# A spectral mixer with two feed-forward layers on one core: the layers run one after the other over all tokens, and layer 2's first product takes two token tiles together as seven block products

## The chip, the core and the metric

The kernel runs on one core of one Trainium2 chip. The metric is the device time of one execution in microseconds (us); less is better. TensorE (PE) multiplies matrices, PEld is its weight load; VectorE (DVE), ScalarE (ACT) and GpSimd (POOL) work element by element; SyncE (SP) issues the DMA transfers. Every engine runs its own list of instructions in order, and the lists are tied together by semaphores.

## The reference, cut to what matters

```
X = rfft(x, axis=1)                               # x: 2 x 3008 x 256, float32
Yr, Yi = complex product of X with w_r, w_i, + bias, then shrink by 0.01 towards 0
x = irfft(Yr + 1j*Yi, n=3008).reshape(6016, 256)
h = x @ moe_w_in;   x = (h * cos(h)) @ moe_w_out                  # 256 -> 2048 -> 256
h = x @ moe2_w_in;  out = (h * clip(h + 3, 0, 6) / 6) @ moe2_w_out
```

## The kernel before, in words

The first 190 us are the mixer: the transforms along the sequence as matmuls, with spills to HBM. The rest, about 1030 us, are the two feed-forward layers. 6016 tokens are 12 tiles: tile 0 has 384 tokens, the others 512. A tile is held as [128, 2, tokens]: two blocks of 128 features. The 2048 hidden features are taken as 8 pairs of two blocks of 128. One step G is one tile and one pair.

Every product is made of three matmuls, since TensorE reads rounded operands: high part of the weights by high part of the data, low by high, high by low. The high part is a rounding copy (`xh`, `gah`, `gbh`, `w1h`), the low part the difference (`xl`, `gal`, `gbl`, `w_lo`). So the first product of a step (`up`, L587) is 2 output blocks x 2 input blocks x 3 = 12 matmuls into two PSUM banks, and the second (`down`, L639) is 12 more, added up over the 8 pairs in two other banks.

Between the two, in layer 1, stands a chain of seven instructions on [128, 2, tokens], i.e. 1024 elements a partition: ACT `phase` (turns, L806), DVE `phase` (angle, L987), DVE `phase` (absolute value, a tensor_scalar that reads and writes SBUF, L991), ACT `cosine` (L814), DVE `ga` = h * cosine (L1009), ACT `gah` (L822), POOL `gal` (L1170). In layer 2 it is ACT `ramp` (L851), DVE `gb` (L1062), ACT `gbh` (L866), POOL `gbl` (L1176).

`feed_forward` runs both layers interleaved: step G of layer 1 and step G - 9 of layer 2 stand side by side in every engine's list (`pair`; `Live` says which parts are there), tiles 2 to 9 in a loop. The output of layer 1 goes from PSUM straight into layer 2's operands (`x2h`, `x2l`). On PE the order is up and down of layer 1, then up and down of layer 2, each `down` for the step before. There is one `phase`, one `ga` and one `gb` buffer. DVE splits the next tile's input into high and low part (L968, L973) in the last step of a tile; for tile 1 that is done in steps 5 and 6. The weights of layer 2 come in with the mixer's DMAs and are split in 16 pieces on ACT and POOL during tiles 0 and 1.

## Time and profile before

| | |
|---|---|
| median of 3 runs | 1220.2 us (1219.81 to 1221.41) |
| the profiled execution | 1220.21 us, of which 1218.4 us are the span from its first to its last instruction |
| PE busy | 1201.4 us (99%), 5576 matmuls |
| PEld, DVE, ACT, POOL busy | 1010.2, 605.7, 631.1, 559.9 us |
| granted TensorE clock, mean | 0.997 of full |
| DMA | 49.76 MB, mean 41 GB/s |

The profile page gives busy times by engine, a chain of waits that ended last, and groups of like instructions; the timeline gives single instructions with start, duration, and the idle time ahead of them. Matmuls are pipelined: one begins before the modelled end of the one before, so that their pace is read from start to start.

### The profile page before, as it was taken

The numbers are of one execution on the slowest core, as the hardware profiler recorded it, in microseconds if no ns is written. First come the engines' busy times: TensorE is split into PE (matmuls) and PEld (weight loads), VectorE is DVE, ScalarE is ACT, GpSimd is POOL, SyncE is SP. The second block draws the span as 40 slices with busy tenths as digits, with TensorE's granted clock in tenths as the row PEclk, the third lists the DMA queues.
The fourth block names the chain that finished last, engine by engine and source line by source line (L and its number), as shares of the span: only waits on it lengthen the run. The fifth ranks groups of instructions, "written<-read, shape, count | busy, mean of one in ns | idle before, by whom it ended". The sixth has DMA issues, their size and how long they took to land.

```text
span 1218.4 us, 14608 instructions
## 1 busy us (share of the span) xinstructions
PE 1201.4 (99%) x5576; PEld 1010.2 (83%) x5576; DVE 605.7 (50%) x599; ACT 631.1 (52%) x705; POOL 559.9 (46%) x294
## 2 busy tenths in 40 slices
PE   8999989999999999999999999999999999999998
PEld 8888789788888888888888888888888888888887
DVE  2787737645445435445354344444354454354344
ACT  2677656665544455445555445544455444554443
POOL 2577656675444443444434444344443444434410
PEclk9999989999999999999999999999999999999999
...
GB/s 251 139 247 230 130 137 115 18 1 1 31 1 1 35 1 0 34 0 29 5 0 34 0 0 34 0 0 34 0 0 34 0 0 34 0 1 18 1 18 18
DMA packets 26209, 49.76 MB, mean 41 GB/s; under 512 B 3185, under 2 KB 9969, under 8 KB 26024
## 3 DMA queue, kind: packets, MB, share of 16 engines
...
## 4 chain that ended last, share of the span: by engine, by line
PE 95%; DVE 2%; DMA 1%; ACT 1%; POOL 0%; issue 0%; SPq 0%; DVEq 0%; ACTq 0%
PE banks L587 41%; PE banks L639 41%; PE banks L492 2%; PE banks L507 2%; PE banks L508 2%; PE banks L512 2%; PE banks L565 2%; PE banks L528 1%; PE banks L527 1%; DMA v<-y_spill 1%; PE banks L477 0%; PE banks L543 0%; PE banks L540 0%; PE banks L541 0%; DVE phase L991 0%; DVE ga L1009 0%
## 5 line engine op out<-in xcount | busy, mean ns | idle before, releaser
L1170 POOL TENSOR_TENSOR gal<-ga,gah 128x1024 fp32r<-128x1024 f32 (+1 forms) x93 | 221.6, 2383 | 515.5 <-ACT gah L822 515.5
L987 DVE SCALAR_TENSOR_TENSOR phase<-phase,banks 128x1024 f32<-128x1024 int32 (+1 forms) x96 | 114.9, 1197 | 273.6 <-ACT phase L806 273.6
L1176 POOL TENSOR_TENSOR gbl<-gb,gbh 128x1024 fp32r<-128x1024 f32 (+1 forms) x88 | 206.6, 2348 | 16.6 <-ACT gbh L866 16.6
L814 ACT ACTIVATE cosine<-phase,half_pi 128x1024 f32<-128x1024 f32 (+1 forms) x96 | 109.1, 1136 | 192.7 <-DVE phase L991 192.1
L806 ACT ACTIVATE phase<-banks 128x1024 int32<-128x1024 f32 (+1 forms) x96 | 97.0, 1011 | 155.5 <-PE banks L587 154.9
L1009 DVE TENSOR_TENSOR ga<-banks,cosine 128x1024 f32<-128x1024 f32 (+1 forms) x96 | 115.4, 1202 | 104.9 <-ACT cosine L814 97.2
L1062 DVE SCALAR_TENSOR_TENSOR gb<-ramp,banks 128x1024 f32<-128x1024 f32 (+1 forms) x95 | 113.8, 1198 | 102.0 <-ACT ramp L851 101.9
L851 ACT ACTIVATE ramp<-banks,three 128x1024 f32<-128x1024 f32 (+1 forms) x95 | 104.3, 1098 | 109.0 <-PE banks L587 109.0
L866 ACT ACTIVATE gbh<-gb 128x1024 fp32r<-128x1024 f32 (+1 forms) x95 | 99.2, 1044 | 35.9 <-DVE gb L1062 31.6
L587 PE MATMUL banks<-xl,w1h 128*128 128x512 f32 (+1 forms) x384 | 116.6, 385 | 0.0
L587 PE MATMUL banks<-xh,w_lo 128*128 128x512 f32 (+1 forms) x384 | 116.6, 385 | 0.0
L587 PE MATMUL banks<-xh,w1h 128*128 128x512 f32 (+1 forms) x352 | 107.0, 385 | 0.0
L587 PE MATMUL banks<-x2h,w_lo 128*128 128x512 f32 (+1 forms) x352 | 106.8, 384 | 0.0
L587 PE MATMUL banks<-x2l,w2h 128*128 128x512 f32 (+1 forms) x352 | 106.7, 384 | 0.0
L587 PE MATMUL banks<-x2h,w2h 128*128 128x512 f32 (+1 forms) x352 | 106.7, 384 | 0.0
L822 ACT ACTIVATE gah<-ga 128x1024 fp32r<-128x1024 f32 (+1 forms) x96 | 99.2, 1034 | 10.6 <-DVE ga L1009 10.6
L639 PE MATMUL banks<-gah,w1h 128*128 128x512 f32 (+1 forms) x384 | 101.2, 385 | 1.9 <-ACT gah L822 1.9
L639 PE MATMUL banks<-gal,w1h 128*128 128x512 f32 (+1 forms) x384 | 101.7, 387 | 0.8 <-POOL gal L1170 0.6
L639 PE MATMUL banks<-gah,w_lo 128*128 128x512 f32 (+1 forms) x384 | 101.0, 385 | 0.0
L639 PE MATMUL banks<-gbh,w2h 128*128 128x512 f32 (+1 forms) x380 | 99.9, 385 | 0.0
L639 PE MATMUL banks<-gbh,w_lo 128*128 128x512 f32 (+1 forms) x380 | 99.8, 384 | 0.0
L639 PE MATMUL banks<-gbl,w2h 128*128 128x512 f32 (+1 forms) x380 | 99.8, 384 | 0.0
...
## 6 DMA issues: line engine op xcount, KB each, us to landing
w<-in_w_ff SPq DMA_DIRECT2D x32, 256.0 KB, 5.9
...
y_spill<-y SPq DMA_DIRECT2D x24, 256.0 KB, 2.2
xf<-x_spill SPq DMA_DIRECT2D x11, 512.0 KB, 4.3
...
out_y<-yt SPq DMA_DIRECT2D x10, 512.0 KB, 3.4
...
```

Of the source, the lines that this page charges most:

```text
L587: mm = pe.matmul(o, w[layer][:, at:at + P], a[:, c, 0:w_tok], start=(n == 0 and c == 0), stop=(n == 2 and c == DC - 1))
L639: mm = pe.matmul(bank[:, at_bank + c, 0:w_tok], w[layer][:, at:at + P], a[:, e, 0:w_tok], start=(p == 0 and n == 0 and e == 0), stop=(p == ...
L806: act.activation(phase[:, :, 0:w].bitcast(i32), bank[:, at:at + 2, 0:w], ACT.Copy, scale=1.0 / (2.0 * math.pi)).then_inc(a_turns, 1)
L814: act.activation(cosine[:, :, 0:w], phase[:, :, 0:w], ACT.Sin, bias=half_pi[:, :], scale=-1.0).then_inc(a_cos, 1)
L822: act.activation(gah[p % 2][:, :, 0:w], ga[:, :, 0:w], ACT.Copy).then_inc(a_gh, 1)
L851: act.activation(ramp[:, :, 0:w], bank[:, at:at + 2, 0:w], ACT.Relu, bias=three[:, :]).then_inc(b_ramp, 1)
L866: act.activation(gbh[pb % 2][:, :, 0:w], gb[:, :, 0:w], ACT.Copy).then_inc(b_gh, 1)
L987: dve.scalar_tensor_tensor(out=phase[:, :, 0:w], in0=phase[:, :, 0:w].bitcast(i32), scalar=-2.0 * math.pi, in1=bank[:, at:at + 2, 0:w], op ...
L1009: dve.tensor_tensor(ga[:, :, 0:w], bank[:, at:at + 2, 0:w], cosine[:, :, 0:w], ALU.mult).then_inc(a_g, 1)
L1062: dve.scalar_tensor_tensor(out=gb[:, :, 0:w], in0=ramp[:, :, 0:w], scalar=6.0, in1=bank[:, at:at + 2, 0:w], op0=ALU.min, op1=ALU.mult).the ...
L1170: pool.tensor_tensor(gal[p % 2][:, :, 0:w], ga[:, :, 0:w], gah[p % 2][:, :, 0:w].bitcast(fp32), ALU.subtract).then_inc(a_gl, 1)
L1176: pool.tensor_tensor(gbl[pb % 2][:, :, 0:w], gb[:, :, 0:w], gbh[pb % 2][:, :, 0:w].bitcast(fp32), ALU.subtract).then_inc(b_gl, 1)
```

## The change

Layer 1 now runs over all 12 tiles (96 steps, `up1(G)` followed by `down1(G - 2)`), and writes its output to HBM (`x2_spill`). Then layer 2 runs over 6 duos of two tiles (1024 tokens; the last duo has 2 x 448) and 8 pairs: 48 steps `step2`. There are two `phase` and two `ga` buffers now, and no loops: every step is written out.

In a step of layer 2 the hidden block is a 2x2 matrix of blocks (output block e by token tile), and so are the weights (A) and the data (B). In place of 8 block products there are 7 (`product`, three matmuls each, in order P1, P5, P2, P6, P3, P7, P4), on sums of blocks of the weights (`sum_w2`: S1 to S4, 4 instructions on 128x128 a pair) and of the data (`sum_t`: T1 to T4, 4 instructions on 128 x 512 a duo). P6 and P7 are added into the bank of P1, P3 into the bank of P5. ACT copies intermediate states out of PSUM (`u1`, `u5`, `u2`), and DVE adds them to what stands in a bank (`c11`, `c12`, `c22`). The fourth block, C21, stays in the bank. Ramp, `gb`, `gbh` and `gbl` are done block by block, 512 elements a partition in place of 1024, four of each a step; for three of the four DVE's `gb` has both operands in SBUF. The second product (`down2`) has 24 matmuls a step as before for two tiles. The seven data blocks of a duo are rounded and split (`round_t` on ACT, `t_low` on POOL) during the duo before; those of duo 1 in steps 5 to 7 of duo 0.

The split of the next tile's input in layer 1 moves from DVE to ACT (`round_x`, pair 3) and POOL (`x_low`, pairs 4 and 5), with two buffers. The weights of layer 2 are loaded and split for pairs 0 to 4 in tiles 2 to 6 of layer 1, for pairs 5 to 7 in the first steps of layer 2.

```diff
-STEPS_A = TILES * PAIRS
-LAG_B = PAIRS + 1
+STEPS1 = TILES * PAIRS
+DUOS = -(-TOKENS // (2 * TOK))
+LAST_W = (TOKENS - (DUOS - 1) * 2 * TOK) // 2
+STEPS2 = DUOS * PAIRS
+S1, S2, S4, A11, A12, A22, S3 = (i * P for i in range(7))
+UP2 = 7 * P
+W2COLS = UP2 + 2 * DIM
+EARLY = 5
+B11, B21, T3, B22, T1, T2, T4 = range(7)
...
+            def product(s, to, a, b, start, done):
+                q, p = divmod(s, PAIRS)
+                w = width2(q)
+                for n, (wt, x) in enumerate(((w2h, th), (w2l, th), (w2h, tl))):
+                    mm = pe.matmul(bank[:, to, 0:w], wt[p][:, a:a + P], x[q % 2][:, b, 0:w],
+                                   start=(start and n == 0), stop=(n == 2),
+                                   skip_group_check=not start)
+                mm.then_inc(done, 1)
+
+            def down2(s, i, c):
+                q, p = divmod(s, PAIRS)
+                e, tile = ((0, 0), (0, 1), (1, 1), (1, 0))[i]
+                count = 4 * s + i + 1
+                if c == 0:
+                    pe.wait_ge(b_gh, count)
+                    pe.wait_ge(b_gl, count)
+                if p == 0 and i == 0:
...
+                for n, (wt, a) in enumerate(((w2h, gbh), (w2l, gbh), (w2h, gbl))):
+                    mm = pe.matmul(bank[:, 4 + 2 * tile + c, 0:w], wt[p][:, at:at + P], a[block][:, 0:w],
+                                   start=(p == 0 and e == 0 and n == 0), stop=(p == PAIRS - 1 and e == 1 and n == 2))
+                if p == PAIRS - 1 and e == 1:
...
+            def step2(s):
+                q, p = divmod(s, PAIRS)
+                x = x_bank(s)
                 if p == 0:
-                    pe.wait_ge(xh_ready, t + 1)
-                    pe.wait_ge(xl_ready, t + 1)
-                if isinstance(G, int) and G <= LAG_B:
-                    if G >= 3:
-                        pe.wait_ge(a_g, G - 2)
-                    elif G == 2:
-                        pe.wait_ge(plus_done, GROUPS - 2)
-                        pe.wait_ge(c_copied, GROUPS - 2)
+                    pe.wait_ge(t_hi, 7 * (q + 1))
+                    pe.wait_ge(t_lo, 7 * (q + 1))
+                if q == 0:
+                    pe.wait_ge(w2_hi, 3 * (p + 1))
+                    pe.wait_ge(w2_lo, 2 * (p + 1))
+                    pe.wait_ge(w2_low_out, p + 1)
+                if s == 0:
+                    pe.wait_ge(a_g, STEPS1 - 2)
+                elif s >= 2:
+                    pe.wait_ge(b_g, 4 * (s - 1))
+                product(s, x, A11, B11, True, p1_done)
+                if s == 0:
+                    pe.wait_ge(a_g, STEPS1 - 1)
                 else:
-                    pe.wait_ge(a_g, G)
-                up(0, h_bank(G), p, x_hi(t), xl, step_width(G), a_h)
+                    pe.wait_ge(c12_done, s)
+                product(s, 2, S1, T1, True, p5_done)
+                if s >= 1:
+                    pe.wait_ge(c11_done, s)
+                product(s, 1, A12, B21, True, p2_done)
+                if s == 0:
+                    down1_half(STEPS1 - 2, 0)
+                else:
+                    down2(s - 1, 0, 0)
+                pe.wait_ge(u1_done, s + 1)
+                product(s, x, S2, T2, False, p6_done)
+                if s == 0:
+                    down1_half(STEPS1 - 2, 1)
+                else:
+                    down2(s - 1, 0, 1)
+                pe.wait_ge(u5_done, s + 1)
+                product(s, 2, S4, B22, False, p3_done)
+                if s >= 1:
+                    down2(s - 1, 1, 0)
+                pe.wait_ge(u2_done, s + 1)
+                product(s, x, S3, T3, False, p7_done)
+                if s == 0:
+                    down1_half(STEPS1 - 1, 0)
+                    down1_half(STEPS1 - 1, 1)
+                else:
+                    down2(s - 1, 1, 1)
+                    down2(s - 1, 2, 0)
+                    down2(s - 1, 2, 1)
+                pe.wait_ge(c22_done, s + 1)
+                product(s, x, A22, T4, False, p4_done)
...
+                up1(G)
                 if G == 2:
                     pe.wait_ge(plus_done, GROUPS)
                     pe.wait_ge(c_copied, GROUPS)
-                down_a(G - 2, G - 2)
-            feed_forward(pe, pair, PAIRS)
+                down1(G - 2)
+            for s in range(STEPS2):
+                step2(s)
...
+            for G in range(1, STEPS1 - 1):
+                take_cos(G)
+                take_turns(G + 1)
+                round_ga(G)
+                if G % PAIRS == 0:
+                    copy_x2(G // PAIRS - 1)
+                prepare1(G)
...
+            for s in range(STEPS2):
+                keep_u1(s)
+                keep_u5(s)
+                if s == 0:
+                    round_ga(STEPS1 - 1)
+                else:
+                    round_gb(s - 1, 3)
+                take_ramp(s, 0)
+                keep_u2(s)
+                round_gb(s, 0)
+                prepare2(s)
+                take_ramp(s, 1)
+                take_ramp(s, 2)
+                round_gb(s, 1)
+                round_gb(s, 2)
+                if s == 0:
+                    copy_x2(TILES - 1)
...
-            def take_ga(G, reuse):
+            def take_ga(G):
                 dve.wait_ge(a_cos, G + 1)
-                if reuse:
-                    dve.wait_ge(a_gh, G)
-                    dve.wait_ge(a_gl, G)
-                at, w = h_bank(G), step_width(G)
...
+                    dve.wait_ge(a_gh, G - 1)
+                    dve.wait_ge(a_gl, G - 1)
+                at, w = h_bank(G), width(G // PAIRS)
+                dve.tensor_tensor(ga[G % 2][:, :, 0:w], bank[:, at:at + 2, 0:w], cosine[:, :, 0:w], ALU.mult).then_inc(a_g, 1)
...
+            def take_c11(s):
+                w = width2(s // PAIRS)
+                dve.wait_ge(p2_done, s + 1)
+                dve.wait_ge(u1_done, s + 1)
+                dve.tensor_tensor(c11[:, 0:w], bank[:, 1, 0:w], u1[:, 0:w], ALU.add).then_inc(c11_done, 1)
...
+            def take_gb(s, i):
+                n, w = 4 * s + i, width2(s // PAIRS)
+                dve.wait_ge(b_ramp, n + 1)
+                if n >= G_BUFS:
+                    dve.wait_ge(b_gh, n - G_BUFS + 1)
+                    dve.wait_ge(b_gl, n - G_BUFS + 1)
+                h = (c11[:, 0:w], c12[:, 0:w], c22[:, 0:w], bank[:, x_bank(s), 0:w])[i]
+                dve.scalar_tensor_tensor(out=gb[n % G_BUFS][:, 0:w], in0=ramp[n % G_BUFS][:, 0:w], scalar=6.0,
+                                         in1=h, op0=ALU.min, op1=ALU.mult).then_inc(b_g, 1)
...
+            for G in range(1, STEPS1 - 1):
+                take_ga(G)
                 take_angle(G + 1)
-            feed_forward(dve, pair, PAIRS)
```

The list of DVE in layer 1, in the middle of a tile, before (`cosine_99` and the like are the program's names with buffer numbers):

```order
L987 SCALAR_TENSOR_TENSOR phase_116<-phase_116,banks 128x1024
L991 TENSOR_SCALAR phase_116<-phase_116 128x1024
L1009 TENSOR_TENSOR ga_96<-banks,cosine_99 128x1024
L1055 REGISTER_ALU
L1059 REGISTER_ALU
L1062 SCALAR_TENSOR_TENSOR gb_97<-ramp_129,banks 128x1024
```

And the same place in the changed kernel, two steps, where `ga1` is of the step before `phase0`:

```order
L1164 TENSOR_TENSOR ga1_132<-banks,cosine_102 128x1024
L1142 SCALAR_TENSOR_TENSOR phase0_100<-phase0_100,banks 128x1024
L1146 TENSOR_SCALAR phase0_100<-phase0_100 128x1024
L1164 TENSOR_TENSOR ga0_103<-banks,cosine_102 128x1024
L1142 SCALAR_TENSOR_TENSOR phase1_101<-phase1_101,banks 128x1024
L1146 TENSOR_SCALAR phase1_101<-phase1_101 128x1024
```

The `gb` of layer 2 no longer stands between one step's `ga` and the next step's angle: the angle follows `ga` directly. In the same way ACT's list of layer 1 is now:

```order
L885 ACTIVATE cosine_102<-phase1_101,half_pi_62 128x1024
L877 ACTIVATE phase0_100<-banks 128x1024
L893 ACTIVATE gah1_105<-ga1_132 128x1024
L885 ACTIVATE cosine_102<-phase0_100,half_pi_62 128x1024
L877 ACTIVATE phase1_101<-banks 128x1024
```

where it was, in the same stretch:

```order
L806 ACTIVATE phase_116<-banks 128x1024
L814 ACTIVATE cosine_99<-phase_116,half_pi_62 128x1024
L851 ACTIVATE ramp_129<-banks,three_63 128x1024
L822 ACTIVATE gah0_120<-ga_96 128x1024
L866 ACTIVATE gbh1_125<-gb_97 128x1024
```

The turns of step G + 1 moved from behind to ahead of the rounding `gah` of step G, and the two instructions of layer 2 are gone from between. PE's list in layer 2, before, is one step of one tile:

```order
L587 MATMUL banks<-x2h,w2h 128x512 x2
L587 MATMUL banks<-x2h,w_lo 128x512 x2
L587 MATMUL banks<-x2l,w2h 128x512 x2
L587 MATMUL banks<-x2h,w2h 128x512 x2
L587 MATMUL banks<-x2h,w_lo 128x512 x2
L587 MATMUL banks<-x2l,w2h 128x512 x2
L639 MATMUL banks<-gbh_124,w2h 128x512 x4
L639 MATMUL banks<-gbh_124,w_lo 128x512 x4
L639 MATMUL banks<-gbl_126,w2h 128x512 x4
```

and in the changed kernel, here P2, a `down2` half, P6 and the next half of a step:

```order
L664 MATMUL banks<-th0_130,w2h4_128 128x512
L664 MATMUL banks<-th0_130,w2_4_lo_142 128x512
L664 MATMUL banks<-t0_lo_144,w2h4_128 128x512
L684 MATMUL banks<-gbh4_175,w2h3_127 128x512
L684 MATMUL banks<-gbh4_175,w2_3_lo_140 128x512
L684 MATMUL banks<-gbl4_176,w2h3_127 128x512
L664 MATMUL banks<-th0_130,w2h4_128 128x512
L664 MATMUL banks<-th0_130,w2_4_lo_142 128x512
L664 MATMUL banks<-t0_lo_144,w2h4_128 128x512
L684 MATMUL banks<-gbh4_175,w2h3_127 128x512
L684 MATMUL banks<-gbh4_175,w2_3_lo_140 128x512
L684 MATMUL banks<-gbl4_176,w2h3_127 128x512
```

The products now come in groups of three matmuls, of this step's first product and the last step's second by turns, where 12 stood together.

## Rows read from the trace of the kernel before

**Rows 1.** The page: busy times, and the chain that ended last by engine.

```profile
PE 1201.4 (99%) x5576; PEld 1010.2 (83%) x5576; DVE 605.7 (50%) x599; ACT 631.1 (52%) x705; POOL 559.9 (46%) x294
...
PE 95%; DVE 2%; DMA 1%; ACT 1%; POOL 0%; issue 0%; SPq 0%; DVEq 0%; ACTq 0%
```

**Rows 2.** The chain of waits in order of time: start, duration, what.

```profile
249.14 2.10 PE banks L587 x12
251.24 2.08 PE banks L639 x12
...
350.08 2.72 PE banks L587 x12
```

**Rows 3.** Timeline of PE where tile 1 begins; idle time in brackets.

```profile
213.90 0.98 PE L639 MATMUL banks<-gal,w1h 128*128 128x384 f32 x4
...
220.97 0.98 PE L639 MATMUL banks<-gah,w1h 128*128 128x384 f32 x4 [0.83 <-ACT gah L822]
...
227.07 1.17 PE L639 MATMUL banks<-gah,w1h 128*128 128x512 f32 x4 [0.45 <-ACT gah L822]
...
233.70 0.74 PE L587 MATMUL banks<-yt_lo,w1h 128*128 128x512 f32 x2 [0.93 <-DVE ga L1009]
```

**Rows 4.** Timeline of PE in the mixer: start, duration, what (21 matmuls apart).

```profile
79.88 0.39 PE L507 MATMUL banks<-wmh,uh 128*128 128x512 f32 x1
...
84.64 0.39 PE L507 MATMUL banks<-wmh,uh 128*128 128x512 f32 x1
```

**Rows 5.** Groups by form: busy, mean ns of one, idle before.

```profile
L845 ACT ACTIVATE ramp<-banks,three 128x512 f32<-128x512 f32 x2 | 1.4, 689 | 1.3 <-PE banks L587 1.3
L1075 DVE TENSOR_TENSOR gbl<-gb,gbh 128x512 fp32r<-128x512 f32 x2 | 1.4, 688 | 0.1
L1126 POOL TENSOR_TENSOR w_lo<-w,w1h 128x512 fp32r<-128x512 f32 x5 | 6.3, 1266 | 7.0 <-ACT w1h L754 7.0
```

**Rows 6.** The page's DMA issues: what, count, KB each, median us to landing.

```profile
xf<-x_spill SPq DMA_DIRECT2D x11, 512.0 KB, 4.3
```

**Rows 7.** Timelines of ACT, DVE and POOL in tile 0 and where tile 1 begins.

```profile
198.50 0.56 DVE L991 TENSOR_SCALAR phase<-phase 128x768 int32<-128x768 int32 x1
198.56 2.20 POOL L1170 TENSOR_TENSOR gal<-ga,gah 128x768 fp32r<-128x768 f32 x1 [2.05 <-ACT gah L822]
219.08 0.96 DVE L1009 TENSOR_TENSOR ga<-banks,cosine 128x768 f32<-128x768 f32 x1 [1.83 <-POOL gal L1170]
219.96 1.21 DVE L987 SCALAR_TENSOR_TENSOR phase<-phase,banks 128x1024 f32<-128x1024 int32 x1
220.99 1.84 POOL L1170 TENSOR_TENSOR gal<-ga,gah 128x768 fp32r<-128x768 f32 x1 [0.79 <-ACT gah L822]
221.20 2.18 DVE L991 TENSOR_SCALAR phase<-phase 128x1024 int32<-128x1024 int32 x1
224.61 1.23 DVE L1009 TENSOR_TENSOR ga<-banks,cosine 128x1024 f32<-128x1024 f32 x1 [1.22 <-ACT cosine L814]
225.87 1.06 ACT L822 ACTIVATE gah<-ga 128x1024 fp32r<-128x1024 f32 x1 [0.60 <-DVE ga L1009]
227.00 2.40 POOL L1170 TENSOR_TENSOR gal<-ga,gah 128x1024 fp32r<-128x1024 f32 x1 [2.47 <-ACT gah L822]
```

**Rows 8.** Timeline of all engines, one step of layer 1 in the loop.

```profile
555.18 1.22 DVE L987 SCALAR_TENSOR_TENSOR phase<-phase,banks 128x1024 f32<-128x1024 int32 x1 [3.90 <-ACT phase L806]
556.44 0.69 DVE L991 TENSOR_SCALAR phase<-phase 128x1024 int32<-128x1024 int32 x1
557.17 1.15 ACT L814 ACTIVATE cosine<-phase,half_pi 128x1024 f32<-128x1024 f32 x1 [2.02 <-DVE phase L991]
558.36 1.22 DVE L1009 TENSOR_TENSOR ga<-banks,cosine 128x1024 f32<-128x1024 f32 x1 [1.22 <-ACT cosine L814]
```

**Rows 9.** Stretches: length, busy by engine, granted clock, DMA share, GB/s.

```profile
156.00:158.00 2.00, 2.00 (x9) 2.00 (x10) 0.00 (x0) 0.07 (x1) 1.72 (x2) 0.50 0.36 74
```

**Rows 10.** Timeline of PE: its longest idle time after the start.

```profile
155.86 2.04 PE L565 MATMUL banks<-c2s,v 120*128 120x120 f32 x8 [4.04 <-DMA v<-y_spill]
```

More of the change, by code:

```diff
@@ new lines, in mixer_program @@
+        r = Region(work_at)
+        for p in range(EARLY):
+            w2f[p], w2l[p] = twice(r, f"w2_{p}", [P, W2COLS])
+        tf[0], tl[0] = twice(r, "t0", [P, 7, TOK])
+        assert r.at <= nc.sbuf_usable_end
+        r = Region(w1_at)
+        c11, c12, c22 = r.place("c11", ONE, fp32), r.place("c12", ONE, fp32), r.place("c22", ONE, fp32)
+        u1, u2 = r.place("u1", ONE, fp32), r.place("u2", ONE, fp32)
+        ramp = [r.place(f"ramp{i}", ONE, fp32) for i in range(2)]
+        assert r.at <= w1_at + 4 * PCOLS * 4
@@ L177, in mixer_program @@
+        gbh, gbl = [], []
+        r = Region(u_at)
+        for i in range(RING):
+            at = r if i < RING - 1 else spare
+            gbh.append(at.place(f"gbh{i}", ONE, f32r))
+            gbl.append(at.place(f"gbl{i}", ONE, f32r))
+        assert spare.at <= small_at and r.at <= phase_at + 2 * TOK * 4
+        th[1] = r.place("th1", [P, 7, TOK], f32r)
+        tf[1], tl[1] = twice(r, "t1", [P, 7, TOK])
+        assert r.at <= v_at
         bank = ctx.enter_context(nc.psum_tensor("banks", [P, 8, 512], fp32))
@@ L700, in _ @@
[L700 to L701 removed]
+                    up1(1)
+            for G in range(2, STEPS1):
+                up1(G)
                 if G == 2:
```

955 lines of the change are left out of this document (558 added, 397 removed).

## The prediction

> **What bounds the kernel now.** The page comes first: PE is busy 99% of the span and stands in 95% of the chain that ended last [rows 1]; no other engine is over half busy except ACT at 52%. From 234 us on the chain of waits alternates 12 matmuls of L587 and 12 of L639 without a gap. So a matmul taken away there is worth its pace, as long as PE is not made to wait. The pace: 12 matmuls of 512 columns take 2.72 us, of 384 columns 2.10 (first product) or 2.08 (second) [rows 2]. That is 0.2267 and 0.1733 to 0.175 us each; a column is (0.2267 - 0.1733)/128 = 0.417 ns, and 448 columns come to 0.200 us. Only the beginning of tile 1 shows feed-forward time lost: between the starts at 213.90 and 233.70 [rows 3] PE issued 36 matmuls of 512 columns and 40 of 384, 8.2 + 6.9 = 15.1 us of work in 19.8 us.
>
> **The change, part by part.**
>
> First product of layer 2. Before: 11 tiles x 8 pairs x 12 = 1056 matmuls at 0.2267 and 96 at 0.175, 256.2 us. After: 21 a step, 40 steps at 0.2267 and 8 steps at 0.200, 190.4 + 33.6 = 224.0 us. **-32.2 us.** The second product: 256.0 before; after 40 x 24 x 0.2267 + 8 x 24 x 0.200 = 256.0. Zero.
>
> The seven waits of a step's products and eight of its second products break PE's list into threes. In the mixer 21 matmuls of mixed lines, with groups of two to six and about as many satisfied waits, go from 79.88 to 84.64 [rows 4], 0.2267 each. A satisfied wait costs nothing; taken at zero, without an upper bound of its own.
>
> Is every wait of a layer-2 step satisfied when PE comes to it? A step is 45 x 0.2267 = 10.20 us, a product 0.68. Half-size work costs 0.69 on ACT and DVE, 1.27 on POOL [rows 5] (copies are nearer 0.6; I take 0.60 to 0.63). Busy: ACT 11 x 0.65 = 7.1, DVE 7 x 0.69 = 4.8, POOL 4 x 1.27 = 5.1. The handoffs, from the step's start, PE's results seen some 0.2 after a group (a matmul's 0.39 less its pace, [rows 4]): u1 0.9 to 1.5, wanted by P6 at 2.72; u5 to 2.2, wanted at 4.08; c11 to 3.0, ramp 3.7, u2 4.3, wanted by P7 at 5.44; c12 5.7, P7 seen at 6.3, c22 7.0, wanted by P4 at 8.16. The least slack is 1.1 us. The low parts are wanted a step later. ACT's roundings for the next duo stand behind these (two a step, 1.3 us, in a hole); the w2 pieces of steps 2 to 4 too. Zero, upper bound in the rivals.
>
> Duo 1 is the exception: POOL has in step 7 four `gbl` and four `t_low`, and step 8 needs all 14 low parts. Counting from step 7: the last `gbl` of step 6 ends at 4.1, then five instructions to 4.1 + 5 x 1.29 = 10.5, against 10.2; with three `gb` of DVE that hold POOL up (below) some 0.5 each, 12.0. **+1.7 us**, from 0.3 to 2.5.
>
> Start of tile 1. The split leaves DVE, comes three pairs ahead, and `w2` pieces no longer stand between. All of 19.8 - 15.1 comes back: **-4.7 us**, from -2 to -5.
>
> Turn from layer 1 to layer 2. The last cosine stands ahead of u1, u5, the last `gah`, ramp and u2 on ACT, and the last `ga` behind c11 on DVE. From the end of the last `up1`: cosine ends at 6.4 (held up as below), u1 at 7.0, where P6 could begin at 6.1; `ga` to 8.9, `gah` 9.95, ramp 10.6, u2 11.2, where P7 could begin at 9.8. **+2.4 us**, from 0.5 to 3.5.
>
> The extra transfers (`x2` out and in again, about 12 MB), the sums for pairs 0 to 4 and duo 0, and `x2` copied by ACT lie under layer 1, whose DMA queue is nearly idle. On SP's queue six loads of w2 for pairs 5 to 7, the last spill of `x2` and the two loads of duo 1 wait for layer 1's end, one behind the other. At 4.3 us for 512 KB [rows 6] pair 5 is there 4 to 9 us later and all of it within 26; DVE asks for pair 5 at the end of step 1, some 10 us later, and for duo 1 at the end of step 4, some 40. Hidden; if pair 5 came 5 us later than this, DVE's c11 would wait in step 2, and PE with it. A tile's end: `x2` is out 1.0 us after the last `down1` is seen, under an `up1` of 2.72. Zero.
>
> **Layer 1 alone, where this is decided.** PE's step is now 24 x 0.2267 = 5.44 us; before it was 10.88, which hid everything. The chain that cannot be doubled up runs from the end of one `ga` to the end of the next. On DVE the angle starts 0.08 before `ga` ends (219.96 against 219.08 + 0.96), and the absolute value 1.24 after the angle's start [rows 7]: 1.16 after `ga`'s end. On the other side `gah` and then `gal`: 227.00 against 225.84, also **1.16** [rows 7]. From the absolute value's start to the end of `ga` are 3.14 us (556.44 to 558.36 + 1.22) [rows 8]. Now the two collide, as twice in [rows 7]. At 198.50 the absolute value started 0.06 first, took its 0.56, and `gal` took 2.20 where alone it takes 1.84. At 220.99 `gal` started 0.21 first, and the absolute value took 2.18 against 0.69 [rows 7, 8] and ended 0.55 after it. One waits for the other's end.
>
> If the absolute value goes first: 1.16 + 3.14 = 4.30 us a step, under 5.44. If `gal` goes first: 1.16 + 2.40 + 0.55 + (3.14 - 0.69) = 6.56 us, over it.
> When the chain is ahead of PE, turns wait for PE; then `gah` follows the turns (they stand ahead of it) and `gal` starts about 0.25 before the absolute value, and wins. That step ends with `ga` 2.0 us after the next step's turns could begin. In the step after that, `gah` waits for `ga`, and the tie of 1.16 decides. Won: `ga` ends 0.9 after PE's time, the chain is ahead again, and the two kinds alternate at PE's pace; the late `gal` ends 11.6 us after its turns began, wanted at 12.5. No wait. Lost: every step of 512 tokens takes 6.56, 88 x 1.12 = +98.6 us. In tile 0 (768 elements) the absolute value leads by 0.06, so it isn't decided there.
> I take it as won. Rows of 0.01 us can't part 1.16 from 1.16; but the angle directly behind `ga` is a bit shorter than after a pause (1.21 [rows 7] against 1.22 [rows 8]), and `gal` is at 1.16 with a `gah` after a pause, as it will be; so the absolute value should be the first by some 0.005 to 0.01.
> The Trainium skill ("SBUF — State Buffer", Who interferes with whom) says that DVE in a two-port mode, or with two inputs in SBUF, and GpSimd take a shared pair of ports as an exclusive lock, and that whoever issues first has it for the whole instruction. On the lock the trace agrees (2.18 against 0.69), and on who gets it too, for leads of 0.06 and 0.21. At 1.16 against 1.16 the rule gives 1187 or 1286 and cannot choose.
>
> **Sum.** Against the span of 1218.4: -32.2 - 4.7 + 1.7 + 2.4 = 1185.6; with the 1.8 us around the span 1187.4. The profiled execution (1220.21) is the median of the runs (1220.2), so no correction: **1187.4 us**. With the bounds of the terms 1184 to 1193.
>
> **Rivals.**
> 1. *The tie is lost* (slower). Place: absolute value L1146 behind `gal` L1344, every step of tiles 1 to 11. It decides as soon as the chain is over 5.44, i.e. when `gal` wins nearly all ties; price +98.6, time 1286. For it: nothing but 0.01 us stands against it, and POOL may ask for its port sooner or later than its start shows. Against it: both rows go to the one that started first. Should PE's idle time of 1.1 us in each step also lower its clock, it is more. The clock fell to 0.50 [rows 9] after idle time of 4.04 us [rows 10]; whether pauses of 1.1 would do it no row shows. I take no loss.
> 2. *Some ties are lost, or layer 2's handoffs miss.* A won tie takes back 1.14 us and a lost one adds 1.12, and `gal` has 0.9 to spare: with a third lost PE waits now and then. Or in layer 2 `gb` with both operands in SBUF collides with `gbl`, 0.3 to 0.5 us each, more than the 1.1 of slack when two meet ahead of u2 or c22; 0.3 us too much in 48 steps are 14 us. Time 1197 to 1217.
> 3. *The start of tile 1 isn't won back and the turns cost their upper bounds*: 1187.4 + 4.7 + 1.9 = 1194. Within the forecast's edge.
> 4. *No change* needs losses of just 32 us: no mechanism gives that but a share of lost ties.
>
> **How the numbers follow.** The forecast (1183 to 1197) gets 0.60, rival 2 0.12, rival 1 0.25, the rest 0.03, most of it between 1217 and 1275. The forecast's own range is 1183 to 1197. As rival 1 alone holds more than 2 in 10, the range reaches to it: 1182 to 1290. A measurement of this kernel tells 0.2% (2.4 us) from no change. Faster: 0.60 + 0.12 + 0.01 = 0.73; within 0.2%: 0.01; slower 0.26.
>
> **What would show it.** 1008 matmuls in `product`, 1152 in the second product, at 0.2267. In layer 1 starts of `up1` 5.44 apart, and durations of the absolute value that alternate between 0.69 and about 2.7; if rival 1 holds, all of them are long, steps are 6.56 apart, and PE waits for `gal`. One idle time of 1 to 2 us where step 8 of layer 2 begins, and two at the turn ahead of P6 and P7. No pause at 213 us. Steps of layer 2 are 10.20 apart. Wrong would be the forecast if the absolute values are all long, or if PE waits for u2 or c22 in the middle of a duo.

## The result, and the profile after

The changed kernel takes **1198.5 us** (median of 4 runs, 1196.6 to 1199.44), the kernel before 1220.3 beside it: a ratio of 0.9818 (95% interval 0.9801 to 0.9835). That is 21.8 us or 1.8% faster. The forecast was 1187.4 us, so 11.1 us too low. The measured time lies in the stated range of 1182 to 1290 only because that range reaches out to rival 1; it is 1.5 us above the forecast's own range (1183 to 1197), and in that of rival 2 (1197 to 1217).

The page of the changed kernel, its busy times and its chain by engine, against [rows 1]:

```profile
PE 1171.4 (98%) x5432; PEld 986.6 (82%) x5432; DVE 790.7 (66%) x839; ACT 777.5 (65%) x1100; POOL 754.2 (63%) x493
...
PE 91%; DVE 3%; DMA 2%; ACT 2%; issue 2%; POOL 0%; SPq 0%; DVEq 0%; ACTq 0%
```

PE is 30 us less busy, but the span is only 20.7 us shorter (1218.4 to 1197.7), and PE's share of the chain fell from 95% to 91%. Part of the gain went into waits.

The place that the prediction called decisive is the pair of the absolute value (DVE, L1146) and `gal` (POOL, L1344). The timeline of the two, two steps late in layer 1, with the idle time ahead in brackets:

```profile
682.11 2.39 POOL L1344 TENSOR_TENSOR gal<-ga,gah 128x1024 fp32r<-128x1024 f32 x1 [1.37 <-ACT gah L893]
682.38 2.68 DVE L1146 TENSOR_SCALAR phase<-phase 128x1024 int32<-128x1024 int32 x1
688.67 0.69 DVE L1146 TENSOR_SCALAR phase<-phase 128x1024 int32<-128x1024 int32 x1
688.68 2.95 POOL L1344 TENSOR_TENSOR gal<-ga,gah 128x1024 fp32r<-128x1024 f32 x1 [4.17 <-ACT gah L893]
```

In one step `gal` starts 0.27 ahead and the absolute value takes 2.68; in the next the absolute value starts 0.01 ahead, takes 0.69, and `gal` takes 2.95. All 88 steps of 512 tokens follow this alternation: 44 ties, each won by DVE with a lead of 9 to 16 ns. PE notices nothing. Its timeline where steps of layer 1 begin shows them 5.44 apart:

```profile
557.47 0.62 PE L625 MATMUL banks<-xh,w1h 128*128 128x512 f32 x2
...
562.91 0.62 PE L625 MATMUL banks<-xh,w1h 128*128 128x512 f32 x2
```

So layer 1 went as predicted. The loss stands in the first duo of layer 2. PE's timeline there: the first matmul of P1 of steps 3, 4, 5, 6, 7 and 8 (727.33, 738.31, 750.66, 765.09, 775.29, 788.28), with the first of P7 in steps 3 to 5 ("issue" means that the profile shows no releaser):

```profile
727.33 0.39 PE L664 MATMUL banks<-th,w2h 128*128 128x512 f32 x1
...
733.41 0.50 PE L664 MATMUL banks<-th,w2h 128*128 128x512 f32 x1 [0.48 <-ACT u L1002]
...
738.31 0.39 PE L664 MATMUL banks<-th,w2h 128*128 128x512 f32 x1
...
745.76 0.50 PE L664 MATMUL banks<-th,w2h 128*128 128x512 f32 x1 [1.85 <-ACT u L1002]
...
750.66 0.39 PE L664 MATMUL banks<-th,w2h 128*128 128x512 f32 x1
...
758.56 0.50 PE L664 MATMUL banks<-th,w2h 128*128 128x512 f32 x1 [2.30 <-ACT u L1002]
...
765.09 0.39 PE L664 MATMUL banks<-th,w2h 128*128 128x512 f32 x1
...
775.29 0.39 PE L664 MATMUL banks<-th,w2h 128*128 128x512 f32 x1
...
788.28 0.47 PE L664 MATMUL banks<-th,w2h 128*128 128x512 f32 x1 [2.63 <-issue]
```

The prediction has 10.20 for a step. Steps 3 to 5 take 10.98, 12.35 and 14.43: 7.2 us more in all, and P7 waits for `u2` (ACT L1002) in each. Step 7 takes 12.99 and step 8 10.28, 2.9 us more, because P1 of step 8 waits (2.63 of idle time; counted from start to start it is 2.8 over the pace). Steps 0 and 1, the turn from layer 1, take 12.51 and 11.15, 3.3 us more. Steps 2 and 6 and all steps 9 to 39 take 10.20.

The timeline of POOL, DVE and ACT around step 4 (begun at 738.31) shows why `u2` is late:

```profile
735.60 2.73 POOL L1366 TENSOR_TENSOR w_lo<-w,w2h 128x448 fp32r<-128x448 f32 x2
736.37 2.51 DVE L1191 SCALAR_TENSOR_TENSOR gb<-ramp,c 128x512 f32<-128x512 f32 x2 [1.27 <-ACT ramp L1017]
...
740.15 0.69 DVE L1191 SCALAR_TENSOR_TENSOR gb<-ramp,banks 128x512 f32<-128x512 f32 x1 [1.27 <-ACT ramp L1017]
740.76 0.68 DVE L1207 TENSOR_TENSOR w<-w 128x128 f32<-128x128 f32 x1
741.47 0.29 DVE L1209 TENSOR_TENSOR w<-w 128x128 f32<-128x128 f32 x1
741.68 0.28 DVE L1210 TENSOR_TENSOR w<-w 128x128 f32<-128x128 f32 x1
742.00 1.26 DVE L1212 TENSOR_TENSOR w<-w 128x128 f32<-128x128 f32 x1
743.19 0.68 DVE L1216 TENSOR_TENSOR w_lo<-w,w2h 128x512 fp32r<-128x512 f32 x1
743.79 0.68 DVE L1170 TENSOR_TENSOR c<-banks,u 128x512 f32<-128x512 f32 x1
744.50 0.72 ACT L1017 ACTIVATE ramp<-c,three 128x512 f32<-128x512 f32 x1 [2.89 <-DVE c L1170]
745.13 0.58 ACT L1002 ACTIVATE u<-banks 128x512 f32<-128x512 f32 x1
```

Five instructions that prepare the weights of later pairs, 3.0 us, stand between `gb` 3 and `c11`. `c11` begins 5.5 us after the step's start, where it begins at 2.24 in steps 9 to 39; ACT's ramp waits 2.89 for it, and `u2` stands behind the ramp. The 3.0 us are not all of it: `gb` 3 itself ends 2.5 after the step's start (0.3 to 1.5 in steps 9 to 39). Ahead of it two `gb` took 2.51 for the pair beside POOL's low parts of w2. In step 2, 1.9 us of DVE's preparation stand at the same place behind a `gb` 3 that ends at 0.4, and `c11` still begins at 2.24.

In step 5 the wait has a second price. Stretches of 3 us each in and behind P7's wait (length, busy by engine, granted clock, DMA share, GB/s):

```profile
755.00:758.00 3.00, 1.26 (x6) 0.72 (x4) 2.16 (x3) 0.70 (x2) 0.32 (x1) 1.00 0.00 0
758.00:761.00 3.00, 2.44 (x7) 1.98 (x8) 1.98 (x3) 2.73 (x7) 1.29 (x1) 0.72 0.00 0
761.00:764.00 3.00, 3.00 (x11) 2.32 (x11) 1.30 (x2) 2.02 (x5) 1.47 (x2) 0.71 0.00 0
```

After the wait of 2.30 the granted clock is 0.72 and 0.71 on average; eight matmuls start 0.43 apart in place of 0.227, i.e. at 1.2 GHz, and cost 1.6 us more. That makes step 5 the longest.

### The profile page after: what moved, and what is told of

Its sections match the earlier page's. It is cut to its first block, busy times and chain, and to the rows that moved or that the text cites. A ratio compares the mean times of both kernels' runs of the same rounds, so it can differ in the third digit from the quotient of the medians.

```text
span 1197.7 us, 15354 instructions
## 1 busy us (share of the span) xinstructions
PE 1171.4 (98%) x5432; PEld 986.6 (82%) x5432; DVE 790.7 (66%) x839; ACT 777.5 (65%) x1100; POOL 754.2 (63%) x493
## 4 chain that ended last, share of the span: by engine, by line
PE 91%; DVE 3%; DMA 2%; ACT 2%; issue 2%; POOL 0%; SPq 0%; DVEq 0%; ACTq 0%
PE banks L625 21%; PE banks L642 21%; PE banks L684 20%; PE banks L664 17%; PE banks L539 2%; PE banks L534 2%; PE banks L535 2%; PE banks L592 1%; PE banks L519 1%; PE banks L555 1%; PE banks L554 1%; DVE gb L1191 1%; DMA xb<-in_x 1%; DMA v<-y_spill 1%; ACT ramp L1017 1%
## 5 line engine op out<-in xcount | busy, mean ns | idle before, releaser
L1344 POOL TENSOR_TENSOR gal<-ga,gah 128x1024 fp32r<-128x1024 f32 (+1 forms) x95 | 249.5, 2626 | 177.8 <-ACT gah L893 176.3
L1424 POOL TENSOR_TENSOR gbl<-gb,gbh 128x512 fp32r<-128x512 f32 (+1 forms) x192 | 248.1, 1304 | 176.0 <-ACT gbh L1024 176.0
L1191 DVE SCALAR_TENSOR_TENSOR gb<-ramp,c 128x512 f32<-128x512 f32 (+1 forms) x144 | 126.1, 881 | 50.9 <-ACT ramp L1017 50.9
L1146 DVE TENSOR_SCALAR phase<-phase 128x1024 int32<-128x1024 int32 (+1 forms) x96 | 156.7, 1632 | 3.3
L1024 ACT ACTIVATE gbh<-gb 128x512 fp32r<-128x512 f32 (+1 forms) x192 | 118.7, 619 | 50.8 <-DVE gb L1191 50.7
L684 PE MATMUL banks<-gbh,w_lo 128*128 128x512 f32 (+1 forms) x384 | 148.6, 387 | 0.0
L664 PE MATMUL banks<-th,w2h 128*128 128x512 f32 (+1 forms) x336 | 130.1, 387 | 9.0 <-ACT u L1002 5.7
L1017 ACT ACTIVATE ramp<-c,three 128x512 f32<-128x512 f32 (+1 forms) x144 | 101.9, 712 | 50.0 <-DVE c L1170 21.1
L664 PE MATMUL banks<-t_lo,w2h 128*128 128x512 f32 (+1 forms) x336 | 129.4, 385 | 0.0
L664 PE MATMUL banks<-th,w_lo 128*128 128x512 f32 (+1 forms) x336 | 129.4, 385 | 0.0
L1142 DVE SCALAR_TENSOR_TENSOR phase<-phase,banks 128x1024 f32<-128x1024 int32 (+1 forms) x96 | 114.6, 1193 | 9.7 <-ACT phase L877 9.7
L625 PE MATMUL banks<-x_lo,w1h 128*128 128x512 f32 (+1 forms) x384 | 116.5, 385 | 0.0
```

Source lines behind the costliest of these rows:

```text
L625: mm = pe.matmul(o, wt[:, at:at + P], a[:, c, 0:w], start=(n == 0 and c == 0), stop=(n == 2 and c == DC - 1))
L664: mm = pe.matmul(bank[:, to, 0:w], wt[p][:, a:a + P], x[q % 2][:, b, 0:w], start=(start and n == 0), stop=(n == 2), skip_group_check=not s ...
L684: mm = pe.matmul(bank[:, 4 + 2 * tile + c, 0:w], wt[p][:, at:at + P], a[block][:, 0:w], start=(p == 0 and e == 0 and n == 0), stop=(p == P ...
L1017: act.activation(ramp[n % G_BUFS][:, 0:w], h, ACT.Relu, bias=three[:, :]).then_inc(b_ramp, 1)
L1024: act.activation(gbh[n % RING][:, 0:w], gb[n % G_BUFS][:, 0:w], ACT.Copy).then_inc(b_gh, 1)
L1142: dve.scalar_tensor_tensor(out=angle[:, :, 0:w], in0=angle[:, :, 0:w].bitcast(i32), scalar=-2.0 * math.pi, in1=bank[:, at:at + 2, 0:w], op ...
```

## The experiments

The times are medians of 4 to 9 runs, in the two runs on the tie of 2; the kernel before had 1220.3 to 1220.4 beside all of them. Steps are those of layer 2 unless said otherwise. "The changed kernel" is the one of the case.

### `u2` ahead of the ramp

```diff
-                take_ramp(s, 0)
                 keep_u2(s)
+                take_ramp(s, 0)
```

> Edit: on ACT, u2 stands ahead of ramp 0 in every step of layer 2 (nothing else moved). Theory A: in steps 3 to 5 of layer 2 P7 waits for u2 because u2 stands behind ramp 0, which waits for c11, and c11 stands on DVE behind the preparation of w2 and of duo 1; those steps lost 0.8 + 2.1 + 4.2 = 7.2 us over 10.20. With u2 first P7 waits for nothing; c22, still late on DVE, holds P4 by some 0.6 and 1.0 us in steps 4 and 5. Steps 3 to 5 lose 1 to 2.5 us in place of 7.2, and the turn to layer 2 gives 0.6 back: about 1193 us (1191 to 1195) against 1198.5 of the changed kernel. Rival B: those steps are bound by ACT or POOL's amount of work (roundings and low parts of w2), so that the order of two instructions moves the loss to another wait: 1197 to 1199.

Measured: 1199.1 us, ratio 0.9828 (0.9814 to 0.9841). No gain. The waits of PE in this kernel, from 690 to 800 us (in total, times, longest):

```profile
PE banks L664 <- ACT u L988: 3.1, 4, 1.0
PE banks L664 <- issue: 3.1, 1, 3.1
PE banks L664 <- DVE c L1182: 2.1, 2, 1.3
...
PE banks L664 <- ACT u L1002: 0.5, 1, 0.5
```

`u2` (L1002) now costs 0.5, at the turn alone, where it cost 5.7. But P4 waits for `c22` (L1182) in steps 4 and 5, P6 for `u1` (L988) in steps 4, 5 and 7, and P1 of step 8 waits longer. Steps 4, 5 and 7 take 12.3, 12.8 and 14.8. The low clock stands elsewhere here: it did not fall in step 5 but behind the wait ahead of step 8 (0.63 from 787 to 790), which took 11.91. Rival B's time and its moved waits held. Its reason, the amount of ACT's or POOL's work, did not: the next run moves only DVE's work, and most of the loss goes. Another order on ACT only changes which product meets the late `c11`.

### DVE's preparation moved away from `c11`

```diff
                 take_c22(s)
+                prepare2(s)
                 take_gb(s, 1)
...
                 take_gb(s, 3)
-                prepare2(s)
```

> Edit: DVE's preparation in layer 2 (sums and low parts of w2, sums of the next duo's blocks) moves from behind gb 3, where c11 of the next step stands behind it, to between c22 and gb 1. Theory A (the amount of DVE's work ahead of c11 makes u2 late): c11 of steps 3 to 5 begins 3.0 to 3.6 us after the step's start in place of 4.1 to 5.9, and of the 7.2 us 0.5 to 2.5 are left: about 1193 us. Rival B (POOL's low parts of w2, which hold gb back on the shared port: two gb took 2.51 us in place of 1.30, push gb 3 and c11 late by themselves): about half of the loss stays, 3 to 4 us: 1195 to 1196. Duo 1's stall of 2.8 us at step 8 stays in both, perhaps 0.3 us more.

Measured: 1193.8 us, ratio 0.9782 (0.9769 to 0.9796), as theory A had it. Steps 3, 4 and 5 take 10.20, 11.11 and 11.57: 2.3 of the 7.2 us are left. The same table of PE's waits:

```profile
...
PE banks L664 <- ACT u L988: 2.3, 3, 1.1
PE banks L664 <- ACT u L1002: 1.1, 1, 1.1
...
```

P7's waits in steps 3 to 5 are gone; the remainder is P6's for `u1`, which stands on ACT behind `gbh` 2 and ramp 3. Steps 7 and 8 (2.6 over) and the turn stayed, as both theories had it. With the same instructions in another place, their place ahead of `c11` is shown as the cause of 4.9 of the 7.2 us (steps alone; 1.6 of it is the low clock of step 5, which didn't come). The rest is the lateness of the `gb`: `c11` of steps 4 and 5 still begins 3.6 and 4.0 after the step's start, directly behind `gb` 3.

### The tie, tried with one short instruction

```diff
                 take_ga(G)
+                dve.memset(pause[:, :], 0.0)
                 take_angle(G + 1)
```

> Edit: in layer 1 DVE clears one element a partition between each ga and the next angle, some 0.06 us. In the trace of the changed kernel every second absolute value begins 9 to 16 ns ahead of gal and takes 0.69 us; with the edit it begins after it. Theory (prediction, rival 1): whoever starts first has the port, so every absolute value of 1024 elements takes about 2.7, a step of layer 1 is 6.56 us long in place of 5.44, 88 steps make +98.6 us: about 1297 us (1285 to 1310); more if PE's clock falls with its pauses of 1.1 us. Rival: the lock isn't decided by 0.06 us of order, or the ring has slack: the alternation stays and the time is 1198 to 1200.

Measured: 1199.5 us, ratio 0.9829 (0.9811 to 0.9848). The clearing overlapped with `ga` and moved the absolute value by only some 14 ns. Timeline of one such tie:

```profile
438.35 2.95 POOL L1346 TENSOR_TENSOR gal<-ga,gah 128x1024 fp32r<-128x1024 f32 x1 [2.47 <-ACT gah L894]
...
438.36 0.69 DVE L1147 TENSOR_SCALAR phase<-phase 128x1024 int32<-128x1024 int32 x1
```

The record of `gal` begins first here, and DVE still has the port. The 44 ties lie between 5 ns behind and 3 ns ahead, and DVE won them all. The edit was too small to test the price, and it shows that the margin is larger than the 9 to 16 ns.

### The tie, lost

```diff
                 take_ga(G)
+                for n in range(3):
+                    dve.memset(pause[:, 32 * n:32 * n + 32], 0.0)
                 take_angle(G + 1)
```

> Edit: as in the run with one small clearing, but three clearings of 32 elements a partition stand between ga and the next angle in layer 1. One clearing moved the start of the absolute value by only some 14 ns (44 ties between 5 ns behind gal and 3 ns ahead of it, all still won by DVE: 0.69 us), so it did not test the rule. Three should put it 0.05 to 0.2 us behind gal. Theory (rival 1 of the prediction): from there on gal has the port first in every step of 1024 elements, the absolute value takes 2.7 to 2.9 us, the ring is 6.56 us, 88 x 1.12 = +98.6 us: about 1297 us (1285 to 1310). Rival: the port isn't given by the order of the starts but by something else (DVE wins all ties below 0.1 us): 1198 to 1201 and the alternation stays.

Measured: 1303.3 us, ratio 1.0679 (1.066 to 1.0699). Timeline of DVE and POOL, two steps in a row:

```profile
501.66 2.40 POOL L1347 TENSOR_TENSOR gal<-ga,gah 128x1024 fp32r<-128x1024 f32 x1 [1.79 <-ACT gah L894]
501.73 2.87 DVE L1147 TENSOR_SCALAR phase<-phase 128x1024 int32<-128x1024 int32 x1
...
508.22 2.39 POOL L1347 TENSOR_TENSOR gal<-ga,gah 128x1024 fp32r<-128x1024 f32 x1 [2.60 <-ACT gah L894]
508.30 2.86 DVE L1147 TENSOR_SCALAR phase<-phase 128x1024 int32<-128x1024 int32 x1
```

0.07 behind is enough: `gal` goes first in every step, the absolute value takes 2.87, and the steps are 6.56 apart, the number of the prediction. Layer 2 begins 100 us later (793.7 against 693.5); the turn adds 3.5. So 0.17 us of clearings cost 105 us: rival 1 was real in mechanism and price, and a shift of 0.08 us is enough to get there. The granted clock over layer 1 stayed at 1.00: PE waited in pieces of 0.2 and 0.4 us, and of 0.6 and 1.1 at the ends of tiles. Layer 1 took 99.3 us more against 98.6 in the prediction, but not quite as priced: 4.3 of it stand in tile 0, where the clearings turned the lead of 0.06 into 0.03 behind, and 95.0 in tiles 1 to 11. One of the steps of tile 0 (768 elements, 0.56 us when it goes first):

```profile
200.89 1.84 POOL L1347 TENSOR_TENSOR gal<-ga,gah 128x768 fp32r<-128x768 f32 x1 [3.34 <-ACT gah L894]
200.92 2.23 DVE L1147 TENSOR_SCALAR phase<-phase 128x768 int32<-128x768 int32 x1
```

The Trainium skill ("SBUF — State Buffer", Who interferes with whom) gives the port to whoever issues first. At 0.07 and at 0.03 us this run agrees; at a few ns the records of the run before don't tell who issued first.

### An eighth block product

```diff
+                product(s, 1, A12, B21, True, None)
                 product(s, 1, A12, B21, True, p2_done)
```

> Edit: P2 is computed twice in each step of layer 2 (three matmuls more, eight block products; the result is the same). Theory (price of a block product is its pace, since PE bounds layer 2): 40 x 3 x 0.2267 + 8 x 3 x 0.2027 = 32.1 us more; steps 3 to 5 and the turn have 0.68 us more cover ahead of P7 each and lose some 2.5 us less: +29.5 us, about 1228 us (1226 to 1231), so slower than the kernel before. Rival: PE has hidden slack in layer 2 (engines other than PE set the step), then +10 or less.

Measured: 1224.6 us, ratio 1.0037 (1.0024 to 1.0051): slower than the kernel before, and 26.1 over the changed kernel, less than the 29.5 of the theory. Steps 9 to 39 take 10.88, exactly 0.68 more. But steps 0 to 8 together take 104.7 against 105.1: nine products more cost nothing there. So leaving out the eighth product earned nothing in the first duo of the changed kernel: its 0.68 a step (6.1 us) came back as waits and, for 1.6 us, as the low clock of step 5, which did not come in this run behind a wait of 1.63.

### The turn

```diff
+            keep_u1(0)
             take_cos(STEPS1 - 1)
...
                 if s == 0:
+                    keep_u2(0)
                     round_ga(STEPS1 - 1)
...
+                if s == 0:
+                    copy_x2(TILES - 1)
                 round_gb(s, 1)
                 round_gb(s, 2)
-                if s == 0:
-                    copy_x2(TILES - 1)
```

The usual places of `keep_u1` and `keep_u2` leave out step 0.

> Edit: at the turn from layer 1 to 2, ACT takes u1 of step 0 ahead of the last cosine, u2 of step 0 ahead of the last gah, and the last copy of x2 ahead of gb's roundings. In the changed kernel step 0 was 12.51 and step 1 11.15 us long, 3.3 over 2 x 10.20. Theory (only the order of these three on ACT costs time): P6 of step 0 doesn't wait (-0.7), P7 neither, the last down of layer 1 waits 0.7 for its gal; step 0 is 10.9 to 11.2, step 1 10.2 to 10.5: -2.3 us, about 1196.3. Rival (the chain ga, gah, gal of the last step of layer 1 bounds the turn): step 0 stays at 12 or more and under 1 us is gained.

Measured: 1196.2 us, ratio 0.9798 (0.9783 to 0.9813). Step 0 takes 11.18 and step 1 10.53: 2.0 of 3.3 us are gone. Steps 2 to 8 took 81.3 against 81.4 in all, but with other parts: the clock fell behind a wait of only 1.80 in step 4 (0.53 from 743 to 746), that step took 13.89, and in step 5 `c11` began at 3.2 in place of 5.9, PE waited for nothing and the step took 10.20. The clock fell again behind the wait ahead of step 8. At the turn, what is left is the last `down` of layer 1, as expected:

```profile
701.17 0.72 PE L655 MATMUL banks<-gal,w1h 128*128 128x512 f32 x2 [0.66 <-POOL gal L1348]
```

### The low parts of duo 1 spread on POOL

POOL's list (`prepare2_first` stands ahead of `gbl` 0 of the step, `prepare2` behind it); ACT rounds the blocks a step earlier to match.

```diff
 prepare2_first
                     if p == 6:
-                        t_low(1, B11, 1, 1)
+                        t_low(1, B22, 3, 3)
                     if p == 7:
-                        t_low(1, B21, 4, 4)
+                        t_low(1, T3, 6, 2)
 prepare2
+                    if p == 5:
+                        t_low(1, B11, 1, 1)
+                        t_low(1, T1, 2, 3)
                     if p == 6:
-                        t_low(1, T1, 2, 3)
-                        t_low(1, B22, 3, 3)
+                        t_low(1, B21, 4, 4)
+                        t_low(1, T2, 5, 4)
                     if p == 7:
-                        t_low(1, T2, 5, 4)
-                        t_low(1, T3, 6, 2)
                         t_low(1, T4, 7, 4)
```

> Edit: the seven low parts of duo 1 are spread on POOL over steps 5, 6 and 7 (2, 3, 2 in place of 0, 3, 4), their roundings on ACT over the same steps; nothing else moves. In the changed kernel P1 of step 8 waited 2.8 us. Theory (POOL's four low parts behind three gbl in step 7 are late): the wait of step 8 is 0 to 0.5; POOL's work in steps 5 and 6 holds some gb back, 0 to 0.6 us more there: 1195.5 to 1196.5. Rival (the same work only waits elsewhere, since the low parts lengthen every gb that stands beside them and with it u1 and c11): the loss moves to P6 and P7 of steps 6 and 7, 1197.5 or more.

Measured: 1200.1 us, ratio 0.9829 (0.9814 to 0.9844): no gain. The wait of step 8 fell to 0.4 us, but step 7 takes 14.69. Timeline of POOL in step 7, and of PE where `down2` waits for what stands behind:

```profile
779.67 2.51 POOL L1380 TENSOR_TENSOR t_lo<-t,th 128x512 fp32r<-128x512 f32 x2 [3.86 <-DVE t L1224]
782.14 4.19 POOL L1424 TENSOR_TENSOR gbl<-gb,gbh 128x512 fp32r<-128x512 f32 x3
```

```profile
783.54 0.47 PE L684 MATMUL banks<-gbh,w2h 128*128 128x512 f32 x1 [2.23 <-POOL gbl L1424]
```

Neither theory named this. The low part of B21 is written over its full value, so it must wait until DVE has taken T4 from it, and DVE did that only behind `gb` 3 of step 6. The spread put B21 ahead of that sum: POOL sat idle for 3.86 us with three `gbl` behind, and the clock fell afterwards too. The edit added a wait of its own, so it says nothing against POOL as the cause of the old one.

### Everything moved together

The edits of the second, the turn's and the last experiment, and POOL's two low parts of a w2 pair one behind `gbl` 0 and one behind `gbl` 1. With DVE's sums earlier, B21 waits only 0.7 for T4.

> Edit: DVE's preparation moved to between c22 and gb 1, the three edits of the turn, duo 1 spread, and POOL's two low parts of a w2 pair put one behind gbl 0 and one behind gbl 1. Theory (the losses of steps 0 to 8, 13.3 us over 10.20 each, come from where preparation stands, not from its amount): 2 to 3 us are left, span some 1186, time 1188 us (1186.5 to 1190). Rival (each edit moves its wait to the next product, as u2 first did): 1190 to 1193.

Measured: **1188.8 us** (1187.2 to 1190.8), ratio 0.9738 (0.9725 to 0.9751), the fastest version with a margin over both kernels. PE's waits from 690 to 800 us:

```profile
PE banks L664 <- ACT u L988: 1.2, 2, 0.8
PE banks L655 <- POOL gal L1348: 0.7, 1, 0.7
...
```

Steps 0 to 8 lose 3.7 us in place of 13.3 over 10.20 each (theory: 2 to 3). Which of the joined edits gave how much beyond the first two wasn't separated.

### The eighth product without the waits

> Edit: the version with all preparation moved, and P2 computed twice in each step of layer 2 (eight block products). In the changed kernel the eighth product cost 0.68 us in steps 9 to 39 but nothing in steps 0 to 8, where waits took it up. Theory (those steps hid it only because they waited): with the waits gone down to 3.7 us it costs close to its full 32.1 us; some 1.5 to 3 us of the remaining waits take it up: 1188.8 + 29 to 30.5 = 1218 to 1219.5, the time of the kernel before within 0.2%. Rival: the steps of duo 0 are bound by another engine's amount of work also here, +26 as before: 1215.

Measured: 1217.3 us, ratio 0.9975 (0.9965 to 0.9985), 28.5 over the version without it and 0.7 under the expected. In the profiled executions it is 29.3 more from the first matmul of layer 2 to the last; layer 2 began 1.5 us earlier in this one, half of it won in the mixer and half in the first steps of layer 1, which the edit doesn't touch. PE's one wait from 690 to 820 us:

```profile
PE banks L655 <- POOL gal L1350: 0.5, 1, 0.5
```

Steps 1 to 5 take 10.88 each. Of the 3.7 us that steps 0 to 8 lost, 0.9 are left; the other 2.8 took up the rest of the 32.1. With eight products the new order of the layers is 0.25% faster than the kernel before; nearly all of the gain is the product left out.

### `u1` ahead of ramp 3 in two steps

```diff
+                if s in (4, 5):
+                    keep_u1(s + 1)
                 take_ramp(s, 3)
```

> Edit: the version with all preparation moved, and ACT takes u1 of steps 5 and 6 ahead of ramp 3 of the step before. There P6 waited 0.5 and 1.0 us for u1. Theory: u1 comes 0.57 earlier, P6 of step 5 waits for nothing, that of step 6 for 0.4; ramp 3, gb 3 and with them c11 come 0.6 later, which P7 has in hand: -1.0 us, about 1187.7 (span 1187.2 less what the mixer varies). Rival: c11 comes late instead, P7 waits, no gain.

Measured: 1189.5 us, ratio 0.9748 (0.9734 to 0.9761), no gain; the rival held. P7 of steps 5 and 6 now waits some 0.3 us each, and P6 of step 6 more than before:

```profile
PE banks L664 <- ACT u L988: 1.3, 1, 1.3
```

`u1` still stands behind `gbh` 2, whose `gb` waits for POOL.

### The changed kernel again

> The changed kernel itself, unchanged, on the same chip as the two runs beside it, to tell how far its time and its trace repeat: 1198.5 us (1196.6 to 1199.5); layer 1 at 5.44 us a step with absolute values of 0.69 and 2.68 us by turns, steps 3, 4, 5 and 7 of layer 2 at 11.0, 12.3, 14.4 and 13.0 us if their waits are fixed by the program; the 1.6 us of step 5 that the lower clock took may stand in another step.

Measured: 1199.9 us (1199.05 to 1200.0), ratio 0.9829 (0.9815 to 0.9842). Steps 0 to 7 repeat to 0.03 us, step 5 with its low clock too. Step 8 took 11.94 where it had taken 10.28. The same two stretches behind P1's wait of step 8, here:

```profile
786.00:789.00 3.00, 1.89 (x7) 1.60 (x8) 0.69 (x1) 1.73 (x3) 3.00 (x3) 0.89 0.64 245
789.00:792.00 3.00, 3.00 (x9) 2.28 (x9) 0.93 (x2) 1.84 (x3) 1.78 (x2) 0.54 0.00 0
```

and in the first profile:

```profile
786.00:789.00 3.00, 0.72 (x3) 0.67 (x4) 1.73 (x2) 1.24 (x3) 3.00 (x3) 1.00 0.91 328
789.00:792.00 3.00, 3.00 (x15) 2.46 (x15) 0.70 (x2) 2.39 (x5) 2.56 (x3) 1.00 0.05 13
```

The wait before P1 is the same to 2 ns. Whether the clock falls after it is not fixed by the program, and moves a run by 1.7 us.

## Why the prediction was right or wrong, point by point

The spans differ by 12.1 us (1197.7 against 1185.6). The terms, with what each measured (the differences of the rows add up to 12.4):

| term | predicted | measured |
|---|---|---|
| first product of layer 2 | -32.2 | -32.2 of PE's work; 448 columns +1.0 |
| start of tile 1 | -4.7 | -4.7, and 0.2 lost ahead of it |
| layer 1 alone | 0 | 0 |
| duo 1, steps 7 and 8 | +1.7 | +2.9 |
| turn, steps 0 and 1 | +2.4 | +3.3 |
| steps 3 to 5 | 0 | **+7.2** |
| mixer, end of the program | 0 | +1.0, +0.9 |

**The step that failed** is "Is every wait of a layer-2 step satisfied when PE comes to it?", answered with zero. It holds for steps 9 to 39: the measured waits are none. But for the first duo the prediction counted ACT's roundings ("the w2 pieces of steps 2 to 4 too") and left out DVE's share of the same preparation, four sums and a low part of w2 and the sums of duo 1, 2.6 to 3.6 us a step in steps 3 to 5, right in front of `c11`. It left out POOL's low parts of w2 as well, which lengthen the `gb` on the port. The least slack was given as 1.1 us; the measured `c11` came 1.9 to 3.7 after 2.24. By the prediction's own sign, PE waiting for `u2` in the middle of a duo, the forecast was wrong.

The second experiment shows DVE's preparation as the cause of most. It was not the cause alone: where `gb` 3 is early, as in step 2, or in steps 10 and 18 with 1.8 us of sums for the next duo, the same place costs nothing. How much the `gb` beside POOL's low parts add was not tried by itself; in the run with everything moved, where these low parts are taken apart, steps 3 to 5 lose 0.7 in place of 2.3 (and step 6, into which work for duo 1 moved, 1.1). The first experiment shows that the lateness can't be hidden by ACT's order. Rival 2 was right that work of DVE and POOL lengthens each other: the fourth sum, 0.29 long in step 2, took 1.26 beside a `gbl`. It named the handoffs, and its range holds the measured time, but it put the loss in all 48 steps, and in steps 9 to 39 there is none.

**Layer 1** was right in each part: the alternation, 0.69 against 2.7, the pace of 5.44, DVE ahead by some 0.01. That it was won is what the prediction took, with a chance of 0.25 against. Its reason was a lead of 0.005 to 0.01, and the lead was 0.009 to 0.016; but DVE also won when its record began 0.005 later, so no lead was needed, and the rows of the kernel before could not tell where the margin ends. The lost tie measured +105 in all against +98.6: the ring was sized exactly (6.56), layer 1 took 99.3 more, and the rest came at the turn and in the steps behind it.

**The first product.** Its work fell as computed. Steps 9 to 39 show the full gain and the eighth product returns 0.68 in each. In the first duo the gain of 0.68 a step came back as waits, so the real effect of the scheme in the changed kernel is 26 us, not 32 (1.6 of the difference is the low clock of step 5).

**Mis-sized terms.** Duo 1, 1.2 us more than predicted: POOL's low parts end last, as said (788.18, and P1 begins at 788.28). POOL in step 7, begun at 775.29:

```profile
779.68 1.29 POOL L1380 TENSOR_TENSOR t_lo<-t,th 128x512 fp32r<-128x512 f32 x1
782.27 1.30 POOL L1424 TENSOR_TENSOR gbl<-gb,gbh 128x512 fp32r<-128x512 f32 x1 [1.29 <-ACT gbh L1024]
783.52 4.66 POOL L1380 TENSOR_TENSOR t_lo<-t,th 128x512 fp32r<-128x512 f32 x3
```

The prediction let POOL run through. Instead it sat idle for 1.29, waiting for the `gbh` of step 7's first block, whose `gb` had taken 1.57 beside the first low part. The last `gbl` of step 6 ended 0.3 later than counted, and the hold-ups beside `gb` were smaller (0.8 in three low parts, where 1.5 was added). Redone, the prediction's own sum for this term is 1.8, not 1.7, and its upper bounds add up to 1192, not 1193; neither matters.

The turn: both waits stood where they were named (P6, P7), 2.3 us against 2.4. Step 1 was not considered, where the last copy of `x2` stood on ACT behind two roundings and ahead of `u1`, +0.95. 448 columns have a pace of 0.2027, not the interpolated 0.200: 9.12 us a step of 45 matmuls. The start of layer 1 came 1.0 us later in the mixer, at 178.9 against 177.9; over the kernels of this study it lay between 177.7 and 180.2, though no experiment touches the mixer, so no effect of the change can be told from it. The end is 0.9 longer from the last matmul on (4.6 against 3.7): four copies and four stores of half a tile where two of each stood.

Transfers and tile ends were hidden, as said: PE waits for no DMA in layer 2.
